# Seven half-size block products for the first product of each expert, issued in one piece

## What is computed

```
h = x @ w_in; g = h - tanh(h); x2 = g @ w_out          # 512 -> 2048 -> 512
P = exp(x2 @ w_gate - max); 8 rounds: P normalised by rows, then by columns
for e in range(8):                                      # w1[e]: 512 x 1024, w2[e]: 1024 x 512
    out += P[:, e] * (relu(x2 @ w1[e]) @ w2[e])
```

## Time and profile before

| | |
|---|---|
| median of 3 runs | 1875.97 us (1874.74 to 1876.88) |
| the profiled execution's own time | 1877.22 us |
| its span in the profile | 1875.4 us |
| TensorE busy | 1855.6 us, 8409 matmul records |
| VectorE, ScalarE, GpSimd busy | 615.5, 413.1, 59.9 us |
| mean granted TensorE clock | 0.997 |
| read from HBM | 50.61 MB |

### The profile page before, as it was taken

One profiled execution on the slowest core, in us unless ns is written; L12 is line 12 of the kernel. 1 busy time (PEld: TensorE's weight loads), 2 busy tenths in 40 slices (PEclk: granted clock), 3 DMA queues, 4 the chain that ended last, 5 costly groups with the idle time before them and its releaser, 6 DMA issues.

```text
span 1875.4 us, 20899 instructions
## 1 busy us (share of the span) xinstructions
PE 1855.6 (99%) x8409; PEld 1533.4 (82%) x8409; DVE 615.5 (33%) x1013; ACT 413.1 (22%) x750; POOL 59.9 (3%) x58
## 2 busy tenths in 40 slices
PE   7999999999999999999999999999999999999999
PEld 5888888888888888888888888888888888888887
DVE  6656665621452113211321232123211321142121
ACT  6434344421121112111211121112111211121111
POOL 4200000310000000000000000000000000000000
PEclk9899999999999999999999999999999999999999
DMA  6101101110020002000200020002000200010001
GB/s 230 45 1 45 45 0 51 46 40 1 0 63 29 0 1 63 29 1 0 69 22 1 0 73 18 1 0 74 18 1 0 74 18 1 0 46 23 1 28 45
DMA packets 28231, 56.41 MB, mean 30 GB/s; under 512 B 5104, under 2 KB 5104, under 8 KB 27248
## 3 DMA queue, kind: packets, MB, share of 16 engines
q1 hardware_dynamic: 28144, 55.08, 9.2%
HBM read 50.61 MB, written 4.46 MB: 29 GB/s over the span
## 4 chain that ended last, share of the span: by engine, by line
PE 97%; DVE 1%; issue 1%; ACT 1%; POOL 0%; DVEq 0%; ACTq 0%; POOLq 0%
PE bank L1128 12%; PE bank L1130 12%; PE bank L1129 12%; PE bank L1142 12%; PE bank L1143 12%; PE bank L1144 12%; PE bank L1097 3%; PE bank L1098 3%; PE bank L1099 3%; PE bank L1081 1%; PE bank L1083 1%; PE bank L1082 1%; PE bank L1037 1%; PE bank L1070 1%; PE bank L1173 1%
## 5 line engine op out<-in xcount | busy, mean ns | idle before, releaser
L763 DVE SCALAR_TENSOR_TENSOR hl<-bank,hh 128x512 fp32r<-128x512 f32 x256 | 177.1, 692 | 952.8 <-ACT hh L538 952.8
L1128 PE MATMUL bank<-xh,w1h 128*128 128x512 f32 x1024 | 400.4, 391 | 0.2
L538 ACT ACTIVATE hh<-bank 128x512 fp32r<-128x512 f32 x256 | 153.1, 598 | 1116.2 <-PE bank L1130 1116.2
L1130 PE MATMUL bank<-xh,w1l 128*128 128x512 f32 x1024 | 398.7, 389 | 0.0
L1142 PE MATMUL bank<-w2h,hh 128*128 128x512 f32 x1024 | 398.5, 389 | 0.0
L1129 PE MATMUL bank<-xl,w1h 128*128 128x512 f32 x1024 | 398.5, 389 | 0.0
L1144 PE MATMUL bank<-w2h,hl 128*128 128x512 f32 x1024 | 398.4, 389 | 0.0
L1143 PE MATMUL bank<-w2l,hh 128*128 128x512 f32 x1024 | 398.3, 389 | 0.0
L1128 PEld LDWEIGHTS bank<-xh,w1h 128*128 128x128 f32 x1024 | 192.3, 188 | 40.8 <-issue 1.3
L1130 PEld LDWEIGHTS bank<-xh,w1l 128*128 128x128 f32 x1024 | 192.2, 188 | 40.3
L1142 PEld LDWEIGHTS bank<-w2h,hh 128*128 128x128 f32 x1024 | 192.2, 188 | 40.0
(11 more groups left out here) (129 smaller groups left out, 1372.0 us busy)
## 6 DMA issues: line engine op xcount, KB each, us to landing
st<-w SPq DMA_DIRECT2D x160, 256.0 KB, 2.7
xT<-xT SPq DMA_DIRECT2D x8, 512.0 KB, 8.0
xn<-xn SPq DMA_DIRECT2D x4, 1024.0 KB, 6.0
out<-yacc SPq DMA_DIRECT2D x3, 1024.0 KB, 3.9
out<-yacc SPq DMA_DIRECT2D x5, 256.0 KB, 2.1
sT<-sT SPq DMA_DIRECT2D x2, 128.0 KB, 3.3
wg_raw<-wg SPq DMA_DIRECT2D x1, 16.0 KB, 2.4
```

Of the source, the lines that this page charges most:

```text
L538: nc.scalar.activation(hh[:, f % NH], hpsum[f % NH][:], ACT.Relu).then_inc(s_hh, 1)
L763: v.scalar_tensor_tensor(hl[:, f % NH], hpsum[f % NH][:], 0.0, hh[:, f % NH].bitcast(f32), ALU.max, ALU.subtract).then_inc(s_hs, 1)
L1128: mm(out, w1h[:, f, k, :], xh[:, k, own_rows(c)], start=(k == 0), stop=False)
L1130: last = mm(out, w1l[:, f, k, :], xh[:, k, own_rows(c)], start=False, stop=(k == KT - 1))
```

## The change

**Blocks.** Two hidden blocks (2 x 128), one batch (2 x 256 tokens) and the model width (2 x 256) are taken as 2 x 2 blocks each, and their product is made from seven block products and not eight, with sums of blocks before and after. A stage is one such product: P1 to P7, each 2 x 3 matmuls with 256 moving columns. The seven go into three PSUM banks (a: P1, P2; b: P6, P7, later P3 over P6; c: P4, P5).

**Order.** An expert's hidden width is visited in two halves (visits), each with its half of w1 and w2, and the batches in two pairs: 8 stages per expert for batches 0 and 1, over all experts (`half` 0), and then the same for batches 2 and 3 (`half` 1). So the weights of the experts are loaded and split twice. Of a stage's second product, the 24 `down` matmuls of the stage before follow the seven products in one piece. Output banks are taken out after every second stage. P1 to P7 stand in `stage` in the order P1, P2, P6, P7, P4, P5, P3, and `OPS * n + P7` in a wait means P7's place in that order.

**Factors.** GpSimd makes the sums of the weights' blocks (`w1_pair_sums`) and the low parts of w1 and w2, ScalarE the high parts; both make the sums and parts of the tokens (`token_sums`, `token_lo`), for batches 2 and 3 at the end of the first half. VectorE makes the sums after the products, ScalarE the relu, VectorE the low parts. The state rows use the same factors of w1: blocks B11, T1 = B12 - B11 and so on, four times 6 matmuls of 256 columns per visit in `half` 0.

**Gate.** The logits are made in one piece from the uncut fp32 `acc`, each 128-row block of the model width in its own 32 columns of the array; 17 products with a 0/1 matrix `sel` turn them and add up the four parts.

The core of the diff; the bodies of the parts that only follow in kind are cut.

```diff
+HT = S // 2
+HK = KT // 2
+OPS = 7
+FACTORS = {P1: (A11, B11), P2: (A12, B21), P3: (S4, B22), P4: (A22, T4), P5: (S1, T1), P6: (S2, T2), P7: (S3, T3)}
...
+    def copy1(n):
+        act.wait_ge(s_p, OPS * n + P2)
+        if not isinstance(n, int) or n:
+            act.wait_ge(s_late, n)
+        nc.scalar.copy(prod1[:], apsum[:, 0:HT]).then_inc(s_c1, 1)
...
+    def w1_pair_sums(v, u, p):
...
+        less(t[:, T1], odd[:, 0:HK], even[:, 0:HK], s_wsum)
+        less(t[:, T3], odd[:, HK:KT], odd[:, 0:HK], s_wsum)
+        pool.wait_ge(s_wsum, 4 * m + 1)
+        less(t[:, T2], odd[:, HK:KT], t[:, T1], s_wsum)
+        pool.wait_ge(s_wsum, 4 * m + 3)
+        less(t[:, T4], even[:, HK:KT], t[:, T2], s_wsum)
...
+    def w1_pair_lo(v, u, p):
+        m = 2 * v + p
+        hi, lo = wc[u][:, p, 0], wc[u][:, p, 1]
+        pool.wait_ge(s_wfh, 3 * m + 1)
+        less(lo[:, B11:B22], st1[:, 2 * p].rearrange("p (o k) f -> p o k f", o=2), raw(hi[:, B11:B22]), s_wfs)
+        pool.wait_ge(s_wfh, 3 * m + 2)
+        less(lo[:, B22], st1[:, 2 * p + 1, HK:KT], raw(hi[:, B22]), s_wfs)
+        pool.wait_ge(s_wfh, 3 * m + 3)
+        less(lo[:, T1:OPS], wf[u][:, p, 1, T1:OPS], raw(hi[:, T1:OPS]), s_wfs)
+    def w2_lo(v, f):
+        pool.wait_ge(s_w2h, DENSE_W2 + v * HF + f + 1)
+        less(w2l[:, f], st2[:, f], raw(w2h[:, f]), s_w2)
...
+    def visit(v, u, more=True, late=None):
+        w2_lo(v, 0)
+        w2_lo(v, 1)
+        if late == 3:
+            token_sums(3)
+        if more:
+            w1_pair_sums(v + 1, 1 - u, 0)
+        w2_lo(v, 2)
+        w2_lo(v, 3)
+        if late == 3:
+            token_lo(3)
+        if more:
+            w1_pair_lo(v + 1, 1 - u, 0)
+        if more:
+            w1_pair_sums(v + 1, 1 - u, 1)
+        if late == 2:
+            token_sums(2)
+            token_lo(2)
+        if more:
+            w1_pair_lo(v + 1, 1 - u, 1)
...
+    def stage(x, l, half, extra=None, more=True):
+        n, v, u, part, p = 8 * x + l, 2 * x + l // 4, l // 4, l % 4, l % 2
+        if half == 0 and part == 3:
+            state_hi(v)
+        copy1(n)
+        if part < 2:
+            if isinstance(v, int) and v == 0:
+                act.wait_ge(s_dy, KT * DH * DC)
+            elif part == 0:
+                act.wait_ge(s_dn, 2 * v)
+                act.wait_ge(s_sy, v if half == 0 else 2 * E)
+            else:
+                act.wait_ge(s_y, ST * 2 * v)
+            w2_hi(v, 2 * part)
+            w2_hi(v, 2 * part + 1)
+        if extra == "logits":
+            logits()
+        relu11(x, l)
+        relu_late(n, p)
+        relu12(n, p)
+        if more and part == 0:
+            w1_pair_plain_hi(v + 1, 1 - u, 0)
+        if more and part == 1:
+            w1_pair_sums_hi(v + 1, 1 - u, 0)
+            w1_pair_plain_hi(v + 1, 1 - u, 1)
+        if more and part == 2:
+            w1_pair_sums_hi(v + 1, 1 - u, 1)
+        if half == 0 and part == 1:
+            state_product1(v)
+        if isinstance(extra, tuple):
+            what, c = extra
+            what(c)
...
+    expert(E - 1, 0, {6: (late_plain_hi, 2), 7: (token_sums_hi, 2)})
+    expert(E, 1, {0: (late_plain_hi, 3), 1: (token_sums_hi, 3)})
...
+    def sum2(n):
+        dve.wait_ge(s_p, OPS * n + P7)
+        dve.wait_ge(s_c1, n + 1)
+        v.tensor_tensor(u2[:], bpsum[:, 0:HT], prod1[:], ALU.add).then_inc(s_u2, 1)
+    def hidden11(x, l):
+        pair_free(x, l)
+        v.tensor_tensor(hf[l % 2][:, 0, 0:HT], apsum[:, HT:S], prod1[:], ALU.add).then_inc(s_h11, 1)
+    def sum3(n):
+        dve.wait_ge(s_h11, n + 1)
+        v.tensor_tensor(u3[:], bpsum[:, HT:S], u2[:], ALU.add).then_inc(s_u3, 1)
+    def sum25(n):
+        v.tensor_tensor(u2[:], cpsum[:, HT:S], u2[:], ALU.add).then_inc(s_v, 1)
+    def hidden_late(x, l):
+        n, p = 8 * x + l, l % 2
+        dve.wait_ge(s_p, OPS * n + P5)
+        dve.wait_ge(s_u3, n + 1)
+        v.tensor_tensor(hf[p][:, :, HT:S], cpsum[:].rearrange("p (f n) -> p f n", f=2),
+                        u3[:].unsqueeze(1).broadcast_to([P, 2, HT]), ALU.add).then_inc(s_late, 1)
...
+    def stage(x, l, half, how="gated", states="gated", middle=None, end=None):
+        n, vis, part, p = 8 * x + l, 2 * x + l // 4, l % 4, l % 2
+        first = isinstance(n, int) and n == 0
+        if half == 0 and part == 2:
+            state_odd(vis)
+        if half == 0 and part == 3:
+            state_lo(vis)
+        sum2(n)
+        hidden11(x, l)
+        sum3(n)
+        hidden_late(x, l)
+        sum25(n)
+        lo11(n, p)
+        if half == 0 and part == 2:
+            state_even(vis)
+        if middle is not None:
+            middle()
+        lo_late(n, p)
+        hidden12(n, p)
+        lo12(n, p)
+        if half == 0 and part == 3:
+            outputs_states(vis, states)
+        if l % 2 == 0 and not first:
+            q = 4 * x + l // 2 - 1
+            c = (0 if half == 0 or isinstance(x, int) and x == E and l == 0 else 2) + (l // 2 + 1) % 2
+            outputs(q, c, how)
+        if end is not None:
+            end()
...
+    def product(which, u, cc, p):
+        out = {P1: apsum[:, 0:HT], P2: apsum[:, HT:S], P6: bpsum[:, 0:HT], P7: bpsum[:, HT:S],
+               P4: cpsum[:, 0:HT], P5: cpsum[:, HT:S], P3: bpsum[:, 0:HT]}[which]
+        a, b = FACTORS[which]
+        w, xs, xr = wc[u], xch[cc], xcl[cc]
+        for k in range(HK):
+            mm(out, w[:, p, 0, b, k, :], xs[:, a, k, :], start=(k == 0), stop=False)
+            mm(out, w[:, p, 0, b, k, :], xr[:, a, k, :], start=False, stop=False)
+            last = mm(out, w[:, p, 1, b, k, :], xs[:, a, k, :], start=False, stop=(k == HK - 1))
+        last.then_inc(s_p, 1)
...
+    def stage(x, l, half):
+        n, u, part, cc, p = 8 * x + l, l // 4, l % 4, l // 2 % 2, l % 2
+        vis = 2 * x + u
+        first = isinstance(n, int) and n == 0
+        if cc == 0:
+            pe.wait_ge(s_wfs, 3 * (2 * vis + p + 1))
+        if half and part == 2:
+            pe.wait_ge(s_xfs, 16)
+        if not first:
+            pe.wait_ge(s_h11, n)
+        product(P1, u, cc, p)
+        product(P2, u, cc, p)
+        if not first:
+            pe.wait_ge(s_h12, n)
+        product(P6, u, cc, p)
+        product(P7, u, cc, p)
+        if not first:
+            pe.wait_ge(s_v, n)
+        product(P4, u, cc, p)
+        product(P5, u, cc, p)
+        pe.wait_ge(s_u3, n + 1)
+        product(P3, u, cc, p)
+        before = (x, l - 1) if l else (x - 1, 7)
+        if first:
+            logits()
+        if half == 0 and part == 2:
+            state_up_even(vis, u)
+        if half == 0 and part == 3:
+            state_down(vis)
+        if not first:
+            down_even(*before)
+        if first:
+            turn_logits()
+        else:
+            down_odd(*before)
+        if half == 0 and part == 1:
+            state_up(vis, u)
+        if half == 0 and part == 2:
+            state_turn(vis)
+    def logits():
+        pe.wait_ge(s_wgin, 16)
+        pe.wait_ge(s_dsum, DENSE_SUMS)
+        for b in [B] + list(range(B)):
+            src, n = (acc_s[:], SB) if b == B else (acc[:, b], S)
+            out = lgpsum if b == B else bank[b]
+            for k in range(KT):
+                at = slice(k * LG, (k + 1) * LG)
+                last = mm(out[at, 0:n], wg[:, k, :], src[:, k, :], start=True, stop=True)
+            last.then_inc(s_lg, 1)
     def turn_logits():
-        pe.wait_ge(s_lgc, C + 1)
-        for t in range(TQ):
-            last = nc.tensor.transpose(lgpsum[:, t * 2 * E:(t + 1) * 2 * E], lg_rows[:, t * P:(t + 1) * P],
-                                       ident[0:2 * E, 0:2 * E])
+        pe.wait_ge(s_sel, 1)
+        for t in [ST_TILE] + list(range(ST_TILE)):
+            if t == ST_TILE:
+                pe.wait_ge(s_lgc, 1)
+                src = hs_f[:, 0:SB]
+            else:
+                if t % ST == 0:
+                    pe.wait_ge(s_lgc, 2 + t // ST)
+                src = lg_rows[:, t // ST, t % ST * P:(t % ST + 1) * P]
+            last = mm(lgpsum[:, t * E:(t + 1) * E], src, sel[:], start=True, stop=True)
         last.then_inc(s_lgt, 1)
...
+    pe.wait_ge(s_xfs, 8)
+    for l in range(8):
+        stage(0, l, 0)
+    with pe.Fori(1, E) as x:
+        for l in range(8):
+            stage(x, l, 0)
+    pe.wait_ge(s_xfs, 12)
+    with pe.Fori(E, 2 * E) as x:
+        for l in range(8):
+            stage(x, l, 1)
+    down_even(2 * E - 1, 7)
+    down_odd(2 * E - 1, 7)
```

More of the change, by code:

```diff
@@ L82, in build @@
[L82 to L102, removed]
@@ L154, in build, with region @@
[L154 to L161, removed]
+        def region(at, *tiles):
+            made = []
+            for name, shape, dt in tiles:
+                size = 4
+                for n in shape[1:]:
+                    size *= n
+                made.append(nc.alloc_sbuf_tensor_at(name, shape, dt, offset=at))
+                at += (size + 31) // 32 * 32
+            return made + [at]
@@ L562, in dense @@
```

(43 more changed lines are left out.)

850 lines of the change are left out of this document (447 added, 403 removed).

## The result

The changed kernel takes **1915.74 us** (median of 4 runs, 1914.57 to 1918.77), the kernel before, on the same chip, 1876.39 us (1874.74 to 1876.88). The ratio is 1.0214, 95% interval [1.0196, 1.0231]: slower by 2.1%, well clear of the scatter. The forecast was 1868 us (1833 to 1902). The result is 48 us over the forecast and 14 us over the top of the range.

The account below looks back on a forecast made before the run. TensorE was taken as the bound, by number of matmuls times distance between starts. Terms -51 + 3 + 17 + 9 - 1 + 5 + 11 gave -7 to -8 us, so 1868 us, range 1833 to 1902.

Parts of the forecast that it names:

- Gate and first stages: Gate logits, Sinkhorn rounds and last dense batch: -1 us for the logits and +5 us for the rest.
- +5 us (1 to 12): Eight Sinkhorn rounds handing over to a busy GpSimd, and long GpSimd operations beside the last dense batch.
- +3 (state rows): State rows: 192 matmuls of 512 columns become 384 of 256, +3 us.
- -1 (gate): Gate logits: column tiles of 32, four at once, take 8.0 us, not 9.6; +3 if tiles don't run together.
- Half-size matmuls, 0.120 us (-51): First product: 5376 matmuls of 256 columns, 0.120 us each, replace 3072 `up` matmuls, saving 51 us.
- Rival 1: TensorE: half-size matmuls run at the pace of their loads, 0.112 us, giving 1838 us; chance 0.25.
- The wait before P3 (+17): Each stage: TensorE loses 0.13 us waiting for `sum3` before P3, +17 us over 128 stages.
- Rival 2: Each stage: P3 waits 0.36 us for VectorE's three sums, giving 1897 us; chance 0.20 with its like.
- The lock (+9): Expert stages: VectorE's two-SBUF subtractions, blocked by GpSimd, overrun their room in about 18 of 64 stages, +9 us.
- Rival 3: Expert stages: the VectorE-GpSimd lock costs 0.5 us in 64 stages, 32 us, not 9, giving 1891 us; chance 0.10.
- The middle (+11): Middle of the expert part: waits of 3.2 and 5.0 us for factors of batches 2 and 3, plus 3 us clock.

Follow-up runs that it names:

- experiment 4: The changed kernel with the eight Sinkhorn column sums made on TensorE as a matmul with ones, not on GpSimd: 1868.3 us.
- experiment 1: The changed kernel with each GpSimd reduction over partitions replaced by one `tensor_tensor`, so its gates are wrong: 1869.76 us.
- experiment 6: The changed kernel with P3 moved behind the first two second-product tiles (six matmuls) of the pair before: 1892.18 us.
- Experiment 8: The changed kernel with experiment 4 and experiment 6, plus earlier `token_sums_hi` for batches 2 and 3 and four w2 low halves on VectorE: 1837.29 us.
- experiment 3: The kernel before with a small GpSimd memset ahead of each of its eight column-sum reductions: 1876.69 us (one run).
- experiment 2: The kernel before with a small GpSimd `tensor_tensor` ahead of each of its eight column-sum reductions: 1936.03 us (one run).

## Why the prediction was wrong, step by step

**The step that failed** is in "Gate and first stages": the eight Sinkhorn rounds at "about 2.3 us and a hand-over to a GpSimd that is now busy", put at **+5 us (1 to 12)** together with the last dense batch. The rounds alone cost about 47: experiment 4 takes 47.4 us away (1915.7 to 1868.3), experiment 1 46.0. The term was mis-sized because the wait in it was wrong: the hand-over to GpSimd was taken as short, and in this order it held two idle stretches, 5.8 to 6.6 and 6.8 to 7.7 us. I had counted GpSimd's work as busy time by length (19.6 us of a visit's 42; measured 20.5) and had not asked what a reduction between two subtractions costs. The kernel before has nine reductions in a row, and each of the eight for sums starts within 0.1 us of its `csum`. Its only change of kind lies under 70.6 us of idle time, and so doesn't show:

```profile
454.88 0.38 POOL L429 PARTITION_ALL_REDUCE amax<-gmax  x1 [70.61 <-DVE gmax L825]
...
491.80 0.40 POOL L432 PARTITION_ALL_REDUCE call<-csum  x1 [3.03 <-DVE csum L838]
494.68 0.40 POOL L432 PARTITION_ALL_REDUCE call<-csum  x1 [2.48 <-DVE csum L838]
```

A row that is short in one order was taken as a price for every order. The range's top of 12 us for this step had no row behind it either: no trace showed a reduction between two subtractions, so it had to be left wide, and it wasn't. The other part of the +5, the last dense batch, was there: before the expert part TensorE waits 3.3 us for `acc` (L1343), which it does not in the kernel before.

The Trainium skill did have the warning (GPSIMD Engine Reference, section Instruction dispatch): the first call into a freshly loaded kernel of GpSimd pays a load of its code of approximately 6 us, with no instruction of its own in the profile. The traces here agree in size (5.8 to 6.8 us ahead of a reduction, marked only "issue"). They differ in one thing: the gap recurs at every change, and also on the way back to `tensor_tensor` (6.8 to 7.7 us). Whether it is that load isn't shown. Had I taken that page's 6 us at each of the 14 changes, which the page doesn't say, GpSimd would stand for 84 us (an estimate) in the six stages (64 us) that hold the rounds, and VectorE takes eight results from it there: a rival with a price, where I had none.

**What held.** Without that step the kernel is where the sum put it. The terms +3 (state rows) and -1 (gate) were not measured apart; of the others:
- *Half-size matmuls, 0.120 us (-51).* Right to 1%. Inside a product they start 0.12 us apart in the kernel after:

```profile
1502.71 0.28 PE L1378 MATMUL bank<-token_factors_hi,w_factors 128*128 128x256 f32 x1
1502.83 0.28 PE L1376 MATMUL bank<-token_factors_hi,w_factors 128*128 128x256 f32 x1
1502.95 0.28 PE L1377 MATMUL bank<-token_factors_lo,w_factors 128*128 128x256 f32 x1
...
1503.31 0.39 PE L1376 MATMUL bank<-token_factors_hi,w_factors 128*128 128x256 f32 x1
```

  The last of them is P3's first, which waited. Over a stage of experiment 6, which has no such wait, (10.52 - 24 x 0.2265) / 42 = 0.121, so -45 and not -51. Rival 1 (0.112) is refuted. The rule of the Trainium skill that leads to it (TensorE: Matmul & The Clock Gate, Back-to-back issue gap), columns divided by 2.4 plus 2.5 ns, doesn't hold for these matmuls, each with its own weight load: 109 ns by it, 120 here. The page gives it for a matmul by itself and says that it comes out too low for a stream with few columns, which the prediction left out.
- *The wait before P3 (+17).* The mechanism was right; the size was 0.185 us a stage (+24), as experiment 6 shows. The part that I had too small is the first hand-over: P7's stream ended at 1501.75, and `sum2` started at 1502.04 in the kernel after, 0.29 us later and not 0.20 (by the prediction's own sum 0.22 us a stage, of which 0.185 show in its length); from there the sums ran as worked out, `sum3` ending 1.21 us after `sum2`'s start (1.20 forecast). Rival 2 (0.36 us) is refuted.
- *The lock (+9).* The long subtractions are there: `relu_lo` at L990 takes 677 ns at best, 693 in the median, 1776 at worst. But TensorE didn't wait for them. From 580 us on, in the kernel after, TensorE's loads waited for `sum3` 105 times and never over 0.2 us, and VectorE itself waited for TensorE before each of the 115 `sum2`, 0.71 us at least and 1.55 in all but one:

```profile
PEld bank L1376 <- DVE sum L961: 17.2, 105, 0.2
```

```profile
DVE sum L951 <- PE bank L1378: 418.3, 115, 13.1
```

  So the lock cost 0; the room of 1.9 us in each second stage was enough. Rival 3 is refuted.
- *The middle (+11).* Two gaps for token factors, 6.5 us together (0.6 and 5.9, where I had 3.2 and 5.0), and clock. The stage at the second gap is 19.19 us long in the kernel after, and not 10.70:

```profile
1227.06 0.42 DVE L961 TENSOR_TENSOR sum<-bank,sum 128x256 f32<-128x256 f32 x1
1246.25 0.43 DVE L961 TENSOR_TENSOR sum<-bank,sum 128x256 f32<-128x256 f32 x1
```

  With 0.8 us more in the stage at the first gap that is 9 us. Experiment 8 took 5.8 of them away. (The fall of the clock that the earlier trace rows are read for lies between their two windows: 50.2 to 54 us, granted clock 0.59, TensorE busy for 2.83 of 3.80.)

-51, 17, 9 and 11 make -14; measured -45, 24, 0 and 9 make -12. Errors of 6, 7, 9 and 2 us cancelled, and that is luck. The change cost 39.4 us in all (1915.74 less 1876.39); with +3, -1 and the 3.3 us of the dense batch taken as they stand, 39.4 + 12 - 3 + 1 - 3.3 = 46 us are left for the rounds, as experiments 1 and 4 say. The forecast was lost by the one term that I had thought too small to work out.

## What to carry to other kernels

An engine's queue is priced by its order, not only by its sum: before work is moved to GpSimd between operations of another kind, look in the trace for a row where the two kinds stand side by side with nothing to hide behind, and if there is none, measure it. A round trip that an in-order engine waits for belongs on the path of everything queued behind it. In this kernel the cross-partition sums of eight columns were better off on TensorE: eight of them cost nothing that could be measured there, and 47 us on a GpSimd that also had elementwise work between them.

## What the runs showed of the hardware that was not expected

GpSimd loses 5.8 to 6.8 us from a `tensor_tensor` to a `partition_all_reduce`, and 6.8 to 7.7 us back; nothing from a memset to the reduction (experiment 3; back to the memset any gap is under the 2.4 to 5 us of waiting for `csum`). The time runs beside a wait for a semaphore: in experiment 2 the `tensor_tensor` had to wait 2.4 us for `csum` after each reduction, and its gap is no longer than in the changed kernel, where nothing held it; under 70.6 us of waiting it can't be seen. No transfer in the trace goes with it: queue 8 has 76 packets of instructions in the kernel before and in both variants of it, with 59 us more in one of them. What GpSimd does in that time these traces don't tell.
